# The two channel mixers of a three-stage model on Trainium2: 2x2 block products regrouped to seven, and the up and down matmuls interleaved

## The reference

```
_moe_ref:   h = xt @ U @ V;                     u = x + h.T;  out = u + relu(u @ w_ch1) @ w_ch2   # w_ch1 512 x 2048, rank 32
_moe2_ref:  h = relu(xt @ w_tok1) @ w_tok2;     u = x + h.T;  out = u + relu(u @ w_ch1) @ w_ch2   # w_ch1 512 x 1536, w_tok1 768 x 256
```

## Time and profile before

| | |
|---|---|
| median of the runs | 791.82 us |
| profiled execution | 792.6 us, of which the span 790.7 us |
| TensorE matmul busy | 768.8 us (97%) |
| VectorE, ScalarE, GpSimd busy | 450.1 us (57%), 361.7 us (46%), 136.0 us (17%) |
| attention / mixers | 0 to 269.1 us / 269.1 to 790.7 us |
| DMA | 81.08 MB, mean 103 GB/s |

### The profile page before, as it was taken

One profiled execution on the slowest core, in us unless ns is written; L12 is line 12 of the kernel. 1 busy time (PEld: TensorE's weight loads), 2 busy tenths in 40 slices (PEclk: granted clock), 3 DMA queues, 4 the chain that ended last, 5 costly groups with the idle time before them and its releaser, 6 DMA issues.

```text
span 790.7 us, 12902 instructions
## 1 busy us (share of the span) xinstructions
PE 768.8 (97%) x3997; PEld 659.8 (83%) x3997; DVE 450.1 (57%) x761; ACT 361.7 (46%) x742; POOL 136.0 (17%) x162
## 2 busy tenths in 40 slices
PE   7989999999999889999999999999999999999998
PEld 6878999999999668888888888888888888888886
DVE  4778999999999684333533353334254335334333
ACT  5567888888888533323333233332123233323321
POOL 1351332233228660000300040000300000000000
PEclk9999999999999999999999999999999999999999
DMA  7935354444441223333323323333003333333334
GB/s 246 225 105 134 94 122 103 119 105 119 105 117 33 70 96 101 93 105 83 104 80 106 99 84 110 88 98 106 0 1 107 93 93 94 93 106 84 103 105 173
DMA packets 82840, 81.08 MB, mean 103 GB/s; under 512 B 7296, under 2 KB 69056, under 8 KB 82816
## 3 DMA queue, kind: packets, MB, share of 16 engines
q1 hardware_dynamic: 82816, 80.77, 37.0%
...
## 4 chain that ended last, share of the span: by engine, by line
PE 63%; DVE 2%; ACT 0%; issue 0%
PE bank L998 29%; PE bank L989 29%; PE bank L976 2%; PE bank L957 2%; PE bank L940 1%; DVE kT_hi L1099 1%; DVE x L1117 0%; DVE x L1150 0%; DVE w_lo L1130 0%; DVE uT_lo L1094 0%; DVE w_lo L1089 0%; DVE t L1108 0%; DVE h_lo L1126 0%; ACT qT_hi L1048 0%; ACT h_hi L1067 0%
## 5 line engine op out<-in xcount | busy, mean ns | idle before, releaser
L1126 DVE SCALAR_TENSOR_TENSOR h_lo<-bank,h_hi 128x512 fp32r<-128x512 f32 x84 | 58.1, 692 | 261.8 <-ACT h_hi L1067 261.8
L1067 ACT ACTIVATE h_hi<-bank 128x512 fp32r<-128x512 f32 x84 | 50.2, 598 | 301.4 <-PE bank L989 301.4
L989 PE MATMUL bank<-uT_hi,w_hi 128*128 128x512 f32 x336 | 131.2, 391 | 0.0
L998 PE MATMUL bank<-w_hi,h_hi 128*128 128x512 f32 x336 | 131.1, 390 | 0.0
L989 PE MATMUL bank<-uT_hi,w_lo 128*128 128x512 f32 x336 | 130.8, 389 | 0.0
L989 PE MATMUL bank<-uT_lo,w_hi 128*128 128x512 f32 x336 | 130.8, 389 | 0.0
L998 PE MATMUL bank<-w_hi,h_lo 128*128 128x512 f32 x336 | 130.7, 389 | 0.0
L998 PE MATMUL bank<-w_lo,h_hi 128*128 128x512 f32 x336 | 130.7, 389 | 0.0
L595 DVE TENSOR_TENSOR pT_lo<-back,pT_hi 128x384 fp32r<-128x384 f32 x192 | 98.1, 552 | 6.9 <-ACT pT_hi L496 3.5
L496 ACT ACTIVATE pT_hi<-back 128x384 fp32r<-128x384 f32 x192 | 84.4, 497 | 36.2 <-PE back L740 34.6
L563 DVE TENSOR_REDUCE negmax<-front 128x1 f32<-128x768 f32 x96 | 91.3, 952 | 9.2 <-PE front L639 9.2
...
## 6 DMA issues: line engine op xcount, KB each, us to landing
...
```

What stands on the lines that cost most here:

```text
L989: last = nc.tensor.matmul(hid[par][:, :], w[par][:, kd, :], y[cc % 2][:, kd, :], start=(kd == 0 and m == 0), stop=(kd == KD - 1 and m == 2))
L998: last = nc.tensor.matmul(acc[k][:, :], y[par][:, k * P:(k + 1) * P], w[par][:, :], start=(start and m == 0), stop=(stop and m == 2))
L1067: nc.scalar.activation(h_hi[par][:, :], hid[par][:, :], ACT.Relu).then_inc(h_hi_made, 1)
L1126: nc.vector.scalar_tensor_tensor(out=h_lo[par][:, :], in0=hid[par][:, :], scalar=0.0, in1=h_hi[par][:, :].bitcast(F32), op0=ALU.max, op1=A ...
```

## The change

The tokens of one batch (768) become a chunk, so there are two chunks per layer (cc = 0 to 3) and the hidden features are taken in pairs of blocks (256): 8, 8, 6 and 6 pairs, 28 in all. Within a pair the up product is a 2x2 by 2x2 block product: the 512 inputs in two halves, the 256 features in two halves, the 768 tokens in two halves of 384. Instead of eight block products it forms seven, by the Winograd form of Strassen's scheme: sums of weight blocks (`pair_sums`) times sums of token blocks (`moving_sum`), each product two 128-row steps x 3 split products = 6 matmuls of 384 columns, and then seven additions (`combine`) and a copy (`snapshot`) that put the hidden tile together in SBUF (`h`). The products go in turn through only two PSUM banks (`hid`), since `acc` now holds six; each must be read before the next but one may start.

The sums of weight blocks are made once per pair, in place in `a_raw`: by GpSimd for pairs 0 and 1, by VectorE for the others. The sums of token blocks, and seven high and seven low parts (`moving_high`, `moving_low`, 768 columns each), are made once per chunk, while the chunk's first pair (p = 0) runs. `down` keeps its 12 x 3 matmuls of 512 columns, now in 12 units, each three matmuls, of which two follow each of products 1 to 6 of the next pair; a chunk's last 12 units come between the transposes of the next chunk. Token mixing of layer 2 is woven into chunks 1 and 2 (`MIXED`): `token_first` after products 2 to 6 of pair 0, `token_second` after product 0 of pair 1; x's split for it is now made by ScalarE (`stage_high`) and GpSimd (`stage_low`). All loops are written out. Buffers overlay each other: w_tok1's raw tile lies in `h`, w_tok2's where `bc_hi` and `bc_lo` come. The additions to x after token mixing (chunk 0) or after the last chunk's down (chunks 1 to 3) are made by `settle`, tile by tile among VectorE's work of pair 0.

The diff cut to its core (8 leading spaces taken off; `moving_sum`, `moving_low`, `w2_low`, `h_low`, `moving_high`, `snapshot` and the like are one instruction each, over 768, 768, 512, 768, 768 and 384 columns; `uT_copy` 512, `a_high` 1792, `w2_high` 512, `h_high` 768, `settle` 512):

```diff
+NCH = 2 * B
+npair = [layers[cc // B][0].shape[1] // (2 * P) for cc in range(NCH)]
+pbase = [sum(npair[:cc]) for cc in range(NCH + 1)]
+PRODS, COMBS, RING = 7, 7, 3
+A_SLOT = (0, 1, 5, 2, 4, 6, 3)
+READ_BY = (0, 1, 2, 3, 5, 6, 7)
+BC_SUM = {2: 2, 3: 3, 4: 1, 6: 4}
+UNITS = [(e, k) for e in range(2) for k in range(NT)]
+MIXED = (1, 2)
...
+acc, hid = bank[0:NT], bank[NT:]
...
+snap = V_raw[:, 0:GW]
+V_hi, V_lo = (flat_a(a_hi[1])[:, i * S:(i + 1) * S] for i in range(2))
+t1 = flat_a(a_lo[1])[:, 0:B * DM].rearrange("p (b c) -> p b c", b=B)
+wt2_hi, wt2_lo = (rows(a, 5, 3).rearrange("p (r s) -> p r s", r=NR) for a in (x_hi, x_lo))
+hs_hi, hs_lo = (rows(a, 8, 3).rearrange("p (e s) -> p e s", e=2) for a in (x_hi, x_lo))
+wt1_raw = h[:, :, :].rearrange("p e s -> p (e s)").rearrange("p (t r) -> p t r", t=NT)
...
+bc_block = (block_of(0, 0), block_of(1, 0), tmp1, block_of(0, 1), tmp2, block_of(1, 1), tmp1)
...
+def up_bank(n, q):
+    return hid[(PRODS * n + q) % 2][:, 0:GW]
+def product_read(eng, n, q):
+    if q == 0:
+        eng.wait_ge(snap_done, n + 1)
+    else:
+        eng.wait_ge(comb_done, COMBS * n + READ_BY[q])
...
-            def load(f, par):
-                wait(sp, w1_made, n0 + f - 1)
-                sp.dma_start(w1_raw[par][:, :, :], wa3[:, :, bass.ds(f * P, P)]).then_inc(w1_in[par], 16)
-                wait(sp, w2_made, n0 + f - 1)
-                sp.dma_start(w2_raw[par][:, :], wb[bass.ds(f * P, P), :]).then_inc(w2_in[par], 16)
...
+    def load_pair(n):
+        cc = max(c for c in range(NCH) if pbase[c] <= n)
+        w3 = layers[cc // B][0].rearrange("(k p) f -> p k f", p=P)
+        wait(sp, a_made, 2 * (n - 1))
+        for i in range(2):
+            f0 = (2 * (n - pbase[cc]) + i) * P
+            sp.dma_start(a_raw[n % 2][:, 2 * i:2 * i + 2, :, :].rearrange("p s k c -> p (s k) c"),
+                         w3[:, :, f0:f0 + P]).then_inc(w1_in[n % 2], 16)
+    def load_w2(n):
+        cc = max(c for c in range(NCH) if pbase[c] <= n)
+        for e in range(2):
+            f0 = (2 * (n - pbase[cc]) + e) * P
+            wait(sp, w2_made, 2 * (n - 1) + e + 1)
+            sp.dma_start(w2_raw[e][:, :], layers[cc // B][1][f0:f0 + P, :]).then_inc(w2_in[e], 16)
...
+    load_pair(0)
+    load_pair(1)
+    sp.dma_start(wt1_raw, w_tok1.rearrange("(p t) r -> p t r", t=NT)).then_inc(wt_in[0], 16)
+    sp.dma_start(wt2_raw[:, :, :], w_tok2.rearrange("(n p) s -> p n s", p=P)).then_inc(wt_in[1], 16)
+    sp.wait_ge(tok_mm, B)
+    load_w2(0)
+    for n in range(pbase[NCH]):
+        if n == pbase[NCH - 1] + 1:
+            store(0)
+        if n + 2 < pbase[NCH]:
+            load_pair(n + 2)
+        if n + 1 < pbase[NCH]:
+            load_w2(n + 1)
...
+    def stage_low(m):
+        pool.wait_ge(st_hi_made, m + 1)
+        nc.gpsimd.tensor_tensor(x_lo[:, m % RING, :], tile_of(x, m), x_hi[:, m % RING, :].bitcast(F32),
+                                ALU.subtract).then_inc(st_made, 1)
...
+    pair_sums(0)
...
+    pool.wait_ge(tok_mm, B)
...
+    pair_sums(1)
+    for cc in MIXED:
+        for t in range(NT):
+            stage_low((cc - 1) * NT + t)
...
+    def product(cc, p, q):
+        n = pbase[cc] + p
+        if p == 0:
+            pe.wait_ge(bc_made, PRODS * cc + q + 1)
+        if q == 0:
+            pe.wait_ge(a_made, 2 * (n + 1))
+        if p == 0 and q < 2:
+            pe.wait_ge(uT_made, cc * NT + NT - 1 + q)
+        elif q < 2:
+            product_read(pe, n - 1, PRODS - 2 + q)
...
+            product_read(pe, n, q - 2)
+        for kt in range(2):
+            for i, (w, y) in enumerate(((a_hi, bc_hi), (a_hi, bc_lo), (a_lo, bc_hi))):
+                last = nc.tensor.matmul(up_bank(n, q), w[n % 2][:, A_SLOT[q], kt, :], y[:, q, kt, :],
+                                        start=(kt == 0 and i == 0), stop=(kt == 1 and i == 2))
+        last.then_inc(prod_done, 1)
+    def down(cc, p, unit):
+        n, (e, k) = pbase[cc] + p, UNITS[unit]
+        if k == 0:
+            pe.wait_ge(w2_made, 2 * n + e + 1)
+            pe.wait_ge(hs_made, 2 * n + e + 1)
+        start, stop = (p == 0 and e == 0), (p == npair[cc] - 1 and e == 1)
+        if start and k == 0:
+            wait(pe, y_made, cc * NT)
+            pe.wait_ge(u_made, min(cc + 2, NCH) * NT)
+        for i, (y, w) in enumerate(((hs_hi, w2_hi), (hs_hi, w2_lo), (hs_lo, w2_hi))):
+            last = nc.tensor.matmul(acc[k][:, :], y[:, e, k * P:(k + 1) * P], w[n % 2][:, e, :],
+                                start=(start and i == 0), stop=(stop and i == 2))
...
+    for b in range(B):
+        token_first_low(b)
+    for t in range(NT):
+        token_second_low(0, t)
+    for t in range(NT):
+        transpose_u(0, t)
+        if t < NT // 2:
+            token_second_low(1, t)
+    for cc in range(NCH):
+        for p in range(npair[cc]):
+            for q in range(PRODS):
+                product(cc, p, q)
+                if p > 0 and q > 0:
+                    down(cc, p - 1, 2 * q - 2)
+                    down(cc, p - 1, 2 * q - 1)
+                if (cc, p, q) == (0, 0, 1):
+                    for t in range(NT // 2, NT):
+                        token_second_low(1, t)
+                if cc in MIXED and p == 0 and q > 1:
+                    token_first(cc, q - 2)
+                    if q == PRODS - 1:
+                        token_first(cc, NT - 1)
+                if cc in MIXED and p == 1 and q == 0:
+                    for t in range(NT):
+                        token_second(cc, t)
+        more = cc + 1 < NCH
+        for unit in range(len(UNITS)):
+            if more and unit == 0:
+                transpose_u(cc + 1, 0)
+            if more and unit < NT - 1:
+                transpose_u(cc + 1, unit + 1)
+            down(cc, npair[cc] - 1, unit)
...
+            if p == 0:
+                for t in range(NT):
+                    uT_copy(cc, t)
+                    if t == NT // 2 - 1:
+                        moving_high(cc, 0)
+                        moving_high(cc, 1)
+                moving_high(cc, 2)
+                if mixed:
+                    stage_high(cc, 0)
+                moving_high(cc, 3)
+                snapshot(n)
+                moving_high(cc, 4)
+                if mixed:
+                    stage_high(cc, 1)
+                moving_high(cc, 5)
+                if mixed:
+                    stage_high(cc, 2)
+                moving_high(cc, 6)
+                if mixed:
+                    stage_high(cc, 3)
+                a_high(n + 1)
+                if mixed:
+                    stage_high(cc, 4)
+                act.wait_ge(bc_made, PRODS * (cc + 1))
+                for e in range(2):
+                    w2_high(n, e)
+                if mixed:
+                    stage_high(cc, 5)
+            else:
+                snapshot(n)
+                for e in range(2):
+                    w2_high(n, e)
+                if n + 1 < pbase[NCH]:
+                    a_high(n + 1)
+            for e in range(2):
+                h_high(n, e)
+            if mixed and p == 0:
+                for r in range(NR):
+                    t2_high(cc, r)
...
+    def pair_sums(n):
+        raw = a_raw[n % 2]
+        dve.wait_ge(w1_in[n % 2], (n // 2 + 1) * 32)
+        nc.vector.tensor_tensor(raw[:, 4, :, :], raw[:, 2, :, :], raw[:, 3, :, :], ALU.add).then_inc(sums_made, 1)
+        dve.wait_ge(sums_made, 4 * n + 1)
+        nc.vector.tensor_tensor(raw[:, 5, :, :], raw[:, 4, :, :], raw[:, 0, :, :], ALU.subtract).then_inc(sums_made, 1)
+        nc.vector.tensor_tensor(raw[:, 2, :, :], raw[:, 0, :, :], raw[:, 2, :, :], ALU.subtract).then_inc(sums_made, 1)
+        dve.wait_ge(sums_made, 4 * n + 2)
+        nc.vector.tensor_tensor(raw[:, 6, :, :], raw[:, 1, :, :], raw[:, 5, :, :], ALU.subtract).then_inc(sums_made, 1)
+    def a_low(n, part):
+        own = slice(0, 4) if part == 0 else slice(4, PRODS)
+        dve.wait_ge(a_hi_made, n + 1)
+        nc.vector.tensor_tensor(a_lo[n % 2][:, own, :, :], a_raw[n % 2][:, own, :, :],
+                                a_hi[n % 2][:, own, :, :].bitcast(F32), ALU.subtract).then_inc(a_made, 1)
...
+    def combine(n, q, dst, other, made=0):
+        dve.wait_ge(prod_done, PRODS * n + q + 1)
+        if q == 1:
+            dve.wait_ge(snap_done, n + 1)
+        else:
+            wait(dve, comb_done, COMBS * n + made if made else 0)
+        nc.vector.tensor_tensor(dst, up_bank(n, q), other, ALU.add).then_inc(comb_done, 1)
...
+        add_mix(0, t)
+    for part in range(2):
+        a_low(0, part)
+    c11, c12, c21, c22 = (c_block(i, k) for i in range(2) for k in range(2))
+    for cc in range(NCH):
+        mixed = cc in MIXED
+        for p in range(npair[cc]):
+            n = pbase[cc] + p
+            more = n + 1 < pbase[NCH]
+            if p == 0:
+                moving_low(cc, 0)
+                moving_low(cc, 1)
+                dve.wait_ge(uT_made, NT * (cc + 1))
+                down_read(dve, n - 2, 1)
```

(53 more changed lines are left out.)

505 lines of the change are left out of this document (242 added, 263 removed).

## The result

The changed kernel takes **824.19 us** (median of 4 runs, 823.67 to 824.89); the kernel before, run beside it, took 791.98 (4 runs). The ratio is 1.0403, 95% interval 1.0382 to 1.0424: slower by 4%. The forecast was 821.0 with a range of 799 to 841. The profiled execution took 824.66 us, its span is 822.7 (before: 792.6 and 790.7).

A forecast was written before the change was run, and what follows sets the result against it. TensorE, busy 97% of the span, was taken as the bound. Columns -21.2, chunk 3 +9.5, chunks 1 and 2 +13.8, head +20.2 and clock +6.8 sum to +29.1 on 792.6: 821.7, as median 821.0 us, range 799 to 841.

The forecast's parts named there:

- columns: Up product: 1176 matmuls of 384 columns at 0.176 us replace 1008 of 512 at 0.2264, saving 21.2 us.
- head: Start of the mixers: VectorE and GpSimd take turns, TensorE stalls 28.9 us where 8.7 before, +20.2 without the clock.
- the clock: At each of four chunk starts, a 3.4 us drop to half rate loses 1.7 us, +6.8 in all.
- chunk 1, chunk 2: Chunk starts with token mixing: token_second waits for t2_low, lengthened by GpSimd collisions; +6.9 us each without the clock.
- chunk 3: Chunk start without token mixing: TensorE waits for VectorE's longer list in the first pair, +9.5 us without the clock.
- Steady pairs: 24 of 28 pairs: TensorE needs 15.5 us, VectorE 9.9, so no stall; smallest margin 1.5 us.
- A sign that did not come: In four stretches of some 20 us, TensorE busy half or less and VectorE nearly full.
- (a): Rival: collision with GpSimd and the clock cost little at head and chunk starts, +11, 803 us; chance 0.2.
- (b): Rival: 384-column matmuls between 512-column ones are paced by 188 ns weight loads, 14 us more, 835; chance 0.08.
- (c): Rival: slower still, by code loading or a steady pair late by a us, +20, 841 us; chance 0.08.
- (d): Rival: VectorE's first-pair instructions on two-dimensional SBUF pieces run at twice the rate, -11, 781 us; chance 0.07.
- (e): Rival: comes out even, 792 us: (a) with the head's loss halved to 6 and chunk 3's to 5; chance 0.02.

The follow-up runs named there:

- run 5: Changed kernel with 46 unused 384-column matmuls put behind products 3 to 6 of chunk 3's pair 0 and product 0 of its pair 1: 818.8 us.
- run 1: Changed kernel with GpSimd's low halves of x (stage_low) at the starts of chunks 1 and 2 cut to one column: 820.2 us.
- Run 4: Changed kernel with VectorE's moving_low in chunks 1 to 3 cut to one column per block: 822.6 us.
- run 3: Changed kernel with VectorE's weight sums in each chunk's first pair moved from ahead of combine 5 to the list's end: 816.60 us.
- run 2: Changed kernel with GpSimd's four instructions that split w_tok2 cut to one column each: 815.3 us.

## Why the prediction was right

Stall is the stage's length less its unstalled length, the clock's share within it.

| term | predicted | measured |
|---|---|---|
| columns, and the steady pair's length | -21.2 | -19.2 |
| head (with 1.7 for the clock) | +21.9 | +19.4 |
| chunk 1, chunk 2 (with 1.7 each) | +8.6 each | +9.2, +9.3 |
| chunk 3 (with 1.7) | +11.2 | +10.0 |
| attention | 0 | +1.6 |
| end, and what is assigned to nothing | 0 | +1.7 |
| sum, on the spans | +29.1 | +32.0 |

**Columns: the price right, one effect missed.** The up matmuls start 0.175 apart (481.11 to 482.16, six of them), as the 0.176 taken from attention. What was missed is the neighbour. Two products and the down units between them, timeline of TensorE:

```profile
481.11 0.33 PE L1083 MATMUL bank<-bc_hi,a_hi 128*128 128x384 f32 x1
...
482.16 0.39 PE L1097 MATMUL bank<-w_hi,qT_hi 128*128 128x512 f32 x1
...
483.55 0.33 PE L1083 MATMUL bank<-bc_hi,a_hi 128*128 128x384 f32 x1
```

Six down matmuls take 1.39 us, 0.2316 each, for 0.2264 in the earlier trace rows. So the pair is 15.64 for 15.54; times the 20 pairs outside the starts that is 2.0 us. By the Trainium skill's formula ("TensorE: Matmul & The Clock Gate", section "Back-to-back issue gap"), which the prediction set beside its rows, up would have fallen by 26.6; the rows were the better guide.

**Steady pairs: no stall, as walked.** TensorE is busy 100.00 of 100.00, VectorE 66 to 67% (9.9 of 15.5 us was the estimate, 64%).

**Chunk 3: right, step by step.** The walk had 9.5 without the clock, run 5 measured 9.5 with the clock kept full. Counted from the end of the last pair's product 6 (703.09), combine 6 ends at 30.1 us, as walked. The clock's own term was too large here: 0.6, not 1.7.

**Chunks 1 and 2: right, with the clock too small.** 9.2 and 9.3 for 8.6. t2_low ended 35.4 us after the last pair's product 6 (427.45 to 462.83), for 35.5 walked. The collision was priced at 2.5 each, and pair 0 in run 1 showed 2.0. The clock cost more than the 1.7: the 36 matmuls of token_second behind t2_low took 10.8 us (462.94 to 473.74) for 8.2 at full clock, 2.6 more. What the walk didn't say is which part of the list counts. Run 4 showed that six us ahead of the last settle could go for 0.6 in pair 0, and run 3 that the sums behind it count in full.

**Head: right by cause, 2.5 too high.** The walk put the end of pair 1's product 1 at 320.8; it ended at 321.6, from a start 1.6 later. Elapsed are 50.9 us for 22.8 of work: 28.1 stalled, 19.4 more than the 8.7 before, and this includes the clock (0.59 in 290 to 295). Taking turns with GpSimd was the mechanism, and run 2 took 6.4 us of it away.

**Clock: mis-sized, and partly luck.** 1.7 for each of four starts was taken as fixed. In chunk 3 it was 0.6 to 1.9 for the same code (runs 1 and 5), in chunk 1 2.6. That too little in one place and too much in the other nearly cancel is luck; the clock's share in the head was not taken apart.

**A sign that did not come.** TensorE was to be busy half or less in each of the four stretches. Over pair 0 it was busy 12.79 of 18.66 us in the head, 16.14 of 20.23 in chunk 1 and 11.04 of 17.15 in chunk 3, though less in single stretches of 5 us. Work at half clock counts as busy nearly twice as long (at a granted clock of 0.50 matmuls of 512 columns started 0.43 us apart in chunk 2, 616.90 to 621.17, at full clock 0.23), and in chunk 1 token_first lies in this stretch. VectorE was nearly full, as foreseen (16.95, 18.14 and 14.80 us).

**What no term held, 1.7.** From the last pair's product 6 to product 0 of the next chunk TensorE took 12.55 us (427.45 to 440.00 and 703.09 to 715.64). 42 matmuls and 24 transposes at the prices of the earlier trace rows are 11.9. Three such passages cost some 2 us.

**Not foreseen:** the attention stage, which the change doesn't touch, was 1.6 us longer in the profiled execution. In 50 to 60 us the granted clock was 0.66 where before it was 0.83 there. Over the nine kernels with the change the mixers started between 267.2 and 272.6, so these runs show no effect of the change in it. With one profile of each kernel they don't show either whether it spreads between executions or between kernels; the changed kernel's four times lie within 1.2 us.

**The rivals.** (a) fails on run 1 and on the head. (b) fails on the 0.175 spacing. (c) fails: the steady pairs are on time; the instruction queue's packets rose from 14 to 26, and no wait was found with them; no run kept the loops, so its share by itself stays untested. (d) fails: the 768-column instruction takes 0.95, at the rate that the prediction took. (e) falls with (a).
